# Bucket numbers in HBM for the attention masks of a three-stage kernel

## What is computed

```python
B, H, S, D = 2, 8, 768, 64
q_bits = (einsum('bhsd,dk->bhsk', q, proj) > 0)       # 6 bits, k likewise
q_bucket = sum(q_bits * 2 ** arange(6), axis=-1)
mask = q_bucket[:, :, :, None] == k_bucket[:, :, None, :]
scores = where(mask, scale * q @ k.T, -1e9)
attn = exp(scores - max(scores))
attn = attn / (sum(attn, axis=-1, keepdims=True) + 1e-09)
out = attn @ v
```

## Time and profile before

| | us |
|---|---|
| median of three runs | 756.55 |
| lowest, highest | 755.89, 757.7 |
| the profiled execution, its own time | 757.69 |
| its span in the trace | 755.9 |
| TensorE busy | 713.7 |
| VectorE busy | 440.0 |
| ScalarE busy | 321.3 |
| GpSimd busy | 265.3 |

### The profile page before, as it was taken

How to read it: one execution, slowest core, us unless ns; L and a number is a source line. 1 busy time by engine, 2 the same in 40 slices (tenths; PEclk the granted TensorE clock), 3 DMA queues, 4 the chain that set the end, 5 groups by cost and what they waited for, 6 DMA issues and landing times.

```text
span 755.9 us, 12025 instructions
## 1 busy us (share of the span) xinstructions
PE 713.7 (94%) x3809; PEld 594.4 (79%) x3809; DVE 440.0 (58%) x794; ACT 321.3 (43%) x634; POOL 265.3 (35%) x269
## 2 busy tenths in 40 slices
PE   5989999999999999999999999999983999999995
PEld 2478888888888987888888888888872788778883
DVE  0399999999999966547446555643438421331110
ACT  0077777787787854221222222222313322443221
POOL 1646667667667751007004401700001121112121
PEclk9999999999999999999999999999995999999998
DMA  9821321321233030001100200010116620101010
GB/s 275 255 63 54 95 63 52 93 64 52 56 87 125 1 112 0 1 2 55 56 1 6 105 0 0 1 55 1 56 57 242 230 86 29 56 28 57 28 57 32
DMA packets 22348, 50.80 MB, mean 67 GB/s; under 512 B 3136, under 2 KB 5312, under 8 KB 22304
## 3 DMA queue, kind: packets, MB, share of 16 engines
q1 hardware_dynamic: 19008, 42.34, 17.5%
q0 software_dynamic: 2320, 7.34, 2.9%
q10 hardware_dynamic: 976, 0.56, 0.4%
HBM read 43.95 MB, written 6.55 MB: 67 GB/s over the span
## 4 chain that ended last, share of the span: by engine, by line
PE 85%; DVE 6%; issue 3%; DMA 3%; ACT 1%; SPq 1%; DVEq 0%; POOL 0%; ACTq 0%; POOLq 0%
PE ps L1188 8%; PE ps L1207 7%; PE ps L1352 6%; PE ps L1353 6%; PE ps L1354 6%; PE ps L1334 6%; PE ps L1336 6%; PE ps L1335 6%; PE ps L1221 4%; PE ps L1222 4%; PE ps L1463 3%; PE ps L1465 3%; PE ps L1464 3%; PE ps L1423 3%; PE ps L1425 3%
## 5 line engine op out<-in xcount | busy, mean ns | idle before, releaser
L612 ACT ACTIVATE probs<-ps,neg_max 128x768 f32<-128x768 f32 x96 | 87.0, 907 | 56.0 <-DVE neg_max L821 55.7
L676 ACT ACTIVATE relu<-ps 128x512 f32<-128x512 f32 x48 | 28.7, 598 | 190.5 <-PE ps L1336 190.5
L830 DVE TENSOR_TENSOR pt_lo<-ps,pt_hi 128x384 fp32r<-128x384 f32 x192 | 98.5, 546 | 5.0 <-ACT pt_hi L623 3.0
L623 ACT ACTIVATE pt_hi<-ps 128x384 fp32r<-128x384 f32 x192 | 86.4, 498 | 25.2 <-PE ps L1207 15.1
L1207 PE MATMUL ps<-cst,probs 128*128 128x128 f32 x576 | 92.1, 276 | 1.9 <-DVE pt_lo L830 1.2
L821 DVE TENSOR_REDUCE neg_max<-ps 128x1 f32<-128x768 f32 x96 | 90.5, 944 | 0.0
L1207 PEld LDWEIGHTS ps<-cst,probs 128*128 128x128 f32 x576 | 69.5, 144 | 10.2 <-DVE pt_lo L830 6.7
L1352 PE MATMUL ps<-wo_hi,g_hi 128*128 128x512 f32 x192 | 76.1, 396 | 0.7 <-DVE xt_lo L898 0.7
L1353 PE MATMUL ps<-wo_lo,g_hi 128*128 128x512 f32 x192 | 75.4, 393 | 0.0
L1354 PE MATMUL ps<-wo_hi,g_lo 128*128 128x512 f32 x192 | 75.4, 393 | 0.0
L1334 PE MATMUL ps<-xt_hi,wi_hi 128*128 128x512 f32 x192 | 75.1, 391 | 0.0
(11 more groups left out here) (155 smaller groups left out, 1531.1 us busy)
## 6 DMA issues: line engine op xcount, KB each, us to landing
w_raw<-w SPq DMA_DIRECT2D x16, 512.0 KB, 5.6
raw_k<-kT SPq DMA_DIRECT2D x32, 192.0 KB, 3.2
raw_q<-qT SPq DMA_DIRECT2D x32, 192.0 KB, 3.5
wi_raw<-w_in SPq DMA_DIRECT2D x4, 1024.0 KB, 5.0
wo_raw<-w_out SPq DMA_DIRECT2D x4, 1024.0 KB, 5.2
pair_raw<-qT SPq DMA_DIRECT2D x8, 384.0 KB, 9.0
pair_raw<-kT SPq DMA_DIRECT2D x8, 384.0 KB, 14.7
raw_v<-v SPq DMA_DIRECT2D x16, 192.0 KB, 2.4
```

What stands on the lines that cost most here:

```text
L830: nc.vector.tensor_tensor(pt_lo[c % 2][sl], unit(tt, h).rearrange("p (k q) -> p k q", k=3), pt_hi[c % 2][sl].bitcast(F32), ALU.subtract).t ...
```

## The change

The bucket numbers themselves are now made once and kept in HBM. At the start TensorE multiplies `bits` with the powers of two (`powers`, made on VectorE from the patterns and a row of indices by seven small operations, `prepare`) for three column ranges of q and of k; VectorE copies the results to `bucket_ids` with a factor 1/32 (the patterns sum gives 32 for each one bit's weight); SyncE writes them with three stores to the HBM tensor `buckets`, waits for these, and goes on to its loop.

In the loop a transfer for each head broadcasts the head's q and k numbers to 64 partitions of `bucket_of`, issued between that head's q and k loads and its v load. At tile 4 of each pair but the last, VectorE makes all masks of the next pair with one comparison of `bucket_of` with the partition's own number (`lane`), which gives 1 or 0 for q and for k. It waits for both transfers of the next pair and until `mask_st` has been read. The matmuls and comparisons beside tiles 2, 3, 5, 6, 8 and 9 are gone. GpSimd copies the q half as before and turns 1 and 0 of the k half into 0 and −2^60 on the way. Pair 0 gets its masks as before.

`row_sum` gets a second column that holds 1e-9, and `add_eps` becomes a reduction over the two columns.

```diff
-MASK_TILES = (2, 3, 5, 6, 8, 9)
-MASK_UNITS = len(MASK_TILES)
+MASK_UNITS = 6
+MASK_TILE = 4
+ID_ROWS = 32
...
+    buckets = nc.dram_tensor("buckets", (NH, 2, SEQ), BF16).ap()
...
-        row_sum = sb("row_sum", [P, CHUNKS_PER_PAIR, CHUNK_TILES], F32)
+        row_sum = sb("row_sum", [P, CHUNKS_PER_PAIR, CHUNK_TILES, 2], F32)
...
+            sp.wait_ge(ids_kept, 2)
+            for a in range(3):
+                sp.dma_start(buckets[:, :, MASK_W * a:MASK_W * (a + 1)],
+                             bucket_ids[ID_ROWS * a:ID_ROWS * a + NH, :, :]).then_inc(ids_out, 16)
+            sp.wait_ge(ids_out, 48)
+
+            def load_buckets(i, z):
+
+                sp.wait_ge(masks_staged, i + (MASK_UNITS - 1))
+                sp.dma_start(bucket_of[half(z, True), :, :], buckets[ds(i * 2 + z, 1), :, :].to_broadcast(
+                    [HD, 2, SEQ])).then_inc(ids_in, 16)
+
             with sp.Fori(1, PAIRS) as i:
-                load_heads(i, False)
+                for z in range(2):
+                    load_head(i, z, False)
+                    load_buckets(i, z)
+                    load_v(i, z, False)
...
-                pool.wait_ge(masks_staged, i * MASK_UNITS + MASK_UNITS)
+                pool.wait_ge(masks_staged, i + MASK_UNITS)
                 pool.wait_ge(scores_done, i * TILES_PER_PAIR + (QT * (z + 1) - TILES_PER_PAIR))
                 m = half(z, True)
-                for c, stack in ((0, qb), (1, kb)):
-                    copied(stack[z][m, :], mask_st[m, c, :], 1.0, masks_in, i * 4 + (2 * z + c + 1))
+                copied(qb[z][m, :], mask_st[m, 0, :], 1.0, masks_in, i * 4 + (2 * z + 1))
+                hold()
+                G.tensor_scalar(kb[z][m, :], mask_st[m, 1, :], 1.0, BIG, ALU.subtract,
+                                ALU.mult).then_inc(masks_in, 1)
+                pool.wait_ge(masks_in, i * 4 + (2 * z + 2))
...
-                if tt in MASK_TILES and not last:
-
+                if tt == MASK_TILE and not last:
+
+                    v_.wait_ge(ids_in, i * 32 + 32)
                     v_.wait_ge(masks_in, i * 4 + 4)
-                    m = MASK_TILES.index(tt)
-                    stage_mask(m, slice(0, P), mask_st[:, m // 3, :], beside(z, MASK_W)).then_inc(masks_staged, 1)
+                    nc.vector.tensor_scalar(mask_st[:, :, :], bucket_of[:, :, :], lane[:, :], None,
+                                            ALU.is_equal).then_inc(masks_staged, 1)
...
-                nc.vector.tensor_scalar(row_eps[:, c, :], row_sum[:, c, :], 1e-9, None, ALU.add).then_inc(eps_done, 1)
+                nc.vector.tensor_reduce(row_eps[:, c, :], row_sum[:, c, :, :], AX, ALU.add).then_inc(eps_done, 1)
...
+            def keep_ids(c):
+                v_.wait_ge(ids_turned, c + 1)
+                nc.vector.tensor_scalar(bucket_ids[:, c, :], ps[0:3 * ID_ROWS, 7 - c, 256:512], 1.0 / 32, None,
+                                        ALU.mult).then_inc(ids_kept, 1)
+
             for c, stack in ((0, qb), (1, kb)):
                 units = range(3 * c, 3 * c + 3)
                 for m in units:
                     keep_bits(m)
+                keep_ids(c)
...
+                pe.wait_ge(prepared, 5)
+                for a in range(3):
+                    last_mm = mm(ps[ID_ROWS * a:ID_ROWS * (a + 1), 7 - c, 256:512], powers[:, :],
+                                 bits[:, c, MASK_W * a:MASK_W * (a + 1)], start=True, stop=True)
+                last_mm.then_inc(ids_turned, 1)
...
-                if tt in MASK_TILES and not last:
-                    last_mm = masks(i + 1, MASK_TILES.index(tt), beside(tt % 2, MASK_W))
```

More of the change, by code:

```diff
@@ L125, in program @@
         mask_st = sb("mask_st", [P, 2, SEQ], BF16, 2)
+        bucket_of = sb("bucket_of", [P, 2, SEQ], BF16, 2)
+        bucket_ids = sb("bucket_ids", [3 * ID_ROWS, 2, MASK_W], BF16, 2)
+        powers = sb("powers", [NH * NBITS, ID_ROWS], BF16, 2)
+        lane_hi = sb("lane_hi", [P, 1], F32)
+        lane = sb("lane", [P, 1], F32)
         raw_q = [sb(f"raw_q{z}", [P, SEQ], F32) for z in range(2)]
@@ L263, in program @@
         masks_staged = sem("masks_staged")
+        prepared = sem("prepared")
+        ids_turned = sem("ids_turned")
+        ids_kept = sem("ids_kept")
+        ids_out = sem("ids_out")
+        ids_in = sem("ids_in")
         masks_in = sem("masks_in")
@@ L380, in load_v @@
                     "a p t d -> (a p) t d")).then_inc(v_in[z], 16)
[L382 to L385, removed]
             load_head(0, 0, True)
@@ L612, in exp @@
                 nc.scalar.activation(probs[z][:, :], score_bank(z), ACT.Exp, bias=neg_max[:, z:z + 1],
-                                     accum_out=row_sum[:, c, j:j + 1]).then_inc(exp_done, 1)
+                                     accum_out=row_sum[:, c, j, 0:1]).then_inc(exp_done, 1)
             def round_units(i, tt, first):
@@ L795, in keep_bits, with first_mask_of @@
                                         ALU.is_gt).then_inc(bits_done, 1)
-            def stage_mask(m, part, dst, src):
+            def first_mask_of(m, part, dst, src):
                 col = MASK_W * (m % 3)
@@ L873, in pair, with prepare @@
                             invert(i - 1, c + CHUNKS_PER_PAIR)
+            def prepare(ins, count):
+                ins.then_inc(prepared, 1)
+                v_.wait_ge(prepared, count)
+            heads = patt[:, :].rearrange("p (h b) -> p h b", b=HD)
+            weighed = x_rows[0:NH * NBITS, 0:2, :, :].rearrange("p a t d -> p (a t d)")[:, 0:NH * HD].rearrange(
+                "p (h b) -> p h b", b=HD)
+            prepare(nc.vector.memset(row_sum[:, :, :, 1], 1e-9), 1)
+            prepare(nc.vector.memset(powers[:, :], 0.0), 2)
+            prepare(nc.vector.tensor_tensor(weighed, heads, iota128[0:NH * NBITS, 0:HD].unsqueeze(1).to_broadcast(
+                [NH * NBITS, NH, HD]), ALU.mult), 3)
+            weights = x_rows[0:NH * NBITS, 2, 0, 0:NH]
+            prepare(nc.vector.tensor_reduce(weights, weighed, AX, ALU.add), 4)
+            prepare(nc.vector.tensor_copy(powers[:, 0:NH], weights), 5)
+            prepare(nc.vector.tensor_scalar(lane_hi[:, :], tokid[:, 0:1], float(HD), -float(HD), ALU.is_gt, ALU.mult), 6)
+            prepare(nc.vector.scalar_tensor_tensor(lane[:, :], tokid[:, 0:1], -1.0, lane_hi[:, :], ALU.add, ALU.add), 7)
+            def keep_ids(c):
+                v_.wait_ge(ids_turned, c + 1)
+                nc.vector.tensor_scalar(bucket_ids[:, c, :], ps[0:3 * ID_ROWS, 7 - c, 256:512], 1.0 / 32, None,
+                                        ALU.mult).then_inc(ids_kept, 1)
             for c, stack in ((0, qb), (1, kb)):
@@ L882, in _ @@
                         v_.wait_ge(masks_turned, m + 1)
-                        placed = stage_mask(m, half(z, True), stack[z], first_mask(m))
+                        placed = first_mask_of(m, half(z, True), stack[z], first_mask(m))
                         if z == 1:
@@ L1135, in _, with masks @@
             mm = nc.tensor.matmul
-            def masks(i, m, dst):
-                return mm(dst, patt[:, ds(i * P, P)],
+            def masks(m, dst):
+                return mm(dst, patt[:, 0:P],
                           bits[:, m // 3, MASK_W * (m % 3):MASK_W * (m % 3) + MASK_W], start=True, stop=True)
@@ L1147, in first_masks @@
                     pe.wait_ge(masks_staged, 2)
+                    pe.wait_ge(ids_kept, 1)
                 for m in range(3 * c, 3 * c + 3):
                     pe.wait_ge(bits_done, m + 1)
-                    masks(0, m, first_mask(m)).then_inc(masks_turned, 1)
+                    masks(m, first_mask(m)).then_inc(masks_turned, 1)
+                pe.wait_ge(prepared, 5)
[3 more added lines that the diff above has]
+                last_mm.then_inc(ids_turned, 1)
             pe.wait_ge(projb_in, 16)
@@ L1172, in turn_back, with scores @@
                 return last_mm
-            def scores(i, tt, first, last):
+            def scores(i, tt, first):
                 z, j = divmod(tt, QT)
@@ L1236, in pair @@
                     if tt < TILES_PER_PAIR - 2:
-                        scores(i, tt + 2, first, last_)
+                        scores(i, tt + 2, first)
                     elif not last_:
-                        scores(i + 1, tt + 2 - TILES_PER_PAIR, False, False)
+                        scores(i + 1, tt + 2 - TILES_PER_PAIR, False)
                     c, part = divmod(tt - 4, CHUNK_TILES)
@@ L1255, in pair @@
                         turn_xt(1)
-            scores(0, 0, True, False)
-            scores(0, 1, True, False)
+            scores(0, 0, True)
+            scores(0, 1, True)
             pe.wait_ge(masks_staged, MASK_UNITS)
+            pe.wait_ge(ids_kept, 2)
             pair(0, True, False)
```

## The result

The changed kernel takes 832.63 us (median of four runs, 827.3 to 835.77) against 757.11 us: 1.099 times as long, 95% interval 1.093 to 1.106. The forecast was 803 us, at most 822. Direction and place were right, the size was not: the loss is 75.5 us where 46 were forecast. The profiled execution took 830.55 us, its span 828.7 us; from the 757.69 us of before, that is +72.9 us.

A forecast was written before the change was run, and what follows sets the result against it. Attention was taken as bound by two nearly full engines, TensorE and VectorE. Six longer intervals between pairs (+41.5 us), the start (+5.7) and the end (−1.0) gave +46.2 us: 803 us as a median, range 784 to 822.

The forecast's parts named there:

- The loop and its point: Attention, tile 4: VectorE's comparison waits some 6.5 us for bucket transfers queued behind loads that need split_qk's last piece.
- The rival of transfers in time: Attention pairs: second bucket transfer goes out before the z=1 loads, VectorE never waits; 745 us, chance 0.07.
- The rival without a lower clock: Attention pairs: the wait comes, clock stays up, VectorE's relief covers part; 787 to 794 us, chance 0.24.
- T to the end of split_qk: GpSimd, from the pair's split_v start for z=0 (T) to the end of the last kb copy: 11.94 us.
- Loads and transfer: DMA queue, each pair: four z=1 loads issued, then the bucket transfer in 3.3 us; landed at T + 17.9.
- Rival 3: Bucket transfers: 64 descriptors reading the same 3 KB of HBM are slow, 3 us more each; 830 us, chance 0.08.
- The comparison: VectorE at tile 4: one instruction of 1536 bf16 elements per partition takes 1.0 us, bounds 0.5 and 2.6.
- TensorE resumes 1.7 us after the comparison: Tile 4: x_rows 0.25, maximum 0.86, first half of pt_lo with its signal 0.6 precede TensorE's restart.
- To the next T: Attention pair: from TensorE's restart to the next pair's split_v start on GpSimd takes 14.5 us.
- Clock: TensorE after its stop in each pair: half clock costs 1.5 us, bounds 0 and 2.5.
- Sum of a beat: Attention, one pair of heads: 36.6 us against 29.68 before, +41.5 us over six intervals.
- The start: Before and in pair 0: making and storing bucket numbers, then a 3.3 us wait, move the first T by +5.7 us.

## Why the prediction was right or wrong

- *The loop and its point*: right. The wait stands at tile 4, is released by `bucket_of`, and its release hangs on the last piece of `split_qk`. The rival of transfers in time, at 0.07, did not come; with the transfers put first and the cheap copy the time is 748 to 750 us, where that rival had 745. The rival without a lower clock, at 0.24, was wrong too: the clock fell to 0.50 in the pairs.
- *T to the end of split_qk, 11.94 us*: this is the step that failed most. It was read from the kernel before, and on that very stretch lies `place_masks`, whose copy the change rewrites. "One operation of the same size in place of another: nothing" was wrong by 1.95 us (2776 ns for 830); the chain ends at 126.96, T + 13.90. Why this copy is slower stays open.
- *Loads and transfer*: issued 2.76 us later (2.6 given); landing 4.20 us in this pair, 4.0 at the median, for which I gave 3.3 from rows of 3.4. With the copy: landed at T + 20.9, where the upper bound was 19.1, so VectorE stood 10.3 us and not 5 to 7. Rival 3, the slow broadcast read, named 830 us, the measured time, but by luck: it took 3 us more for a transfer, and a median of 4.0 against 3.3 for the loads of k is an excess of 0.7.
- *The comparison*: 1.0 us given; from landing to `x_rows` it took 1.91 us. The bound of 0.5 to 2.6 held. By itself it takes 0.62 us; two of the seven did so, and the two shortest beats, 38.5 and 39.6 us, are theirs. The Trainium skill, "VectorE: DVE Perf Modes", section "The perf-mode tier table", led to an estimate of 0.56 us: the 0.62 us where nothing holds it up is near it. Behind a GpSimd operation, with up to 2.22 us, it does not hold. The Trainium skill, "GPSIMD Engine Reference", section "Key points", says that GpSimd contends with VectorE instructions in a 2-port mode, which would explain it; I had used that sentence for the reduction only.
- *TensorE resumes 1.7 us after the comparison*: 1.73. *To the next T*: 14.5 given, 14.68 at full clock. *Clock*: 1.5 given, 1.7 measured. All three were right.
- *Sum of a beat*: 36.6 given; 36.6 + 1.95 (copy) + 0.15 (issue) + 0.9 (landing) + 0.9 (comparison) + 0.4 (TensorE and its clock) = 40.9, the pair shown. Over six intervals the mean excess is 40.34 − 36.6 = 3.7, so 22.5 us.
- *The start*: first T at 68.0 given, 72.16 measured, +4.2. "`prepare` runs on an idle VectorE" was wrong. It is idle for want of constants, which come at 21.8 us; then the operations run until 26.5 and the first bits wait, at 26.58 us where VectorE began at 23.70 before. The first line here is of the kernel before, the others are of the changed one:

```profile
23.70 1.08 DVE L793 TENSOR_SCALAR bits<-ps 96x256 bf16<-96x256 f32 x3 [23.70 <-PE ps L1161]
...
21.79 0.07 DVE L909 MEMSET row_sum<- 128x12 f32 x1 [21.79 <-DMA mb_sb<-mod_bias]
...
26.58 1.08 DVE L818 TENSOR_SCALAR bits<-ps 96x256 bf16<-96x256 f32 x3
...
54.21 1.70 DVE L839 TENSOR_SCALAR mask_st<-bucket_of,lane 128x1536 bf16<-128x1536 bf16 x1 [5.91 <-issue]
```

  The bits of k come 1.9 us later than before, at 36.20. The last bucket transfer goes out at 49.28 us (46.5 given), and the comparison starts at 54.21 (49.8 given), 4.9 us behind it where 3.3 was given. So of the 4.2 us 2.8 are lost by the issue, of which `prepare` makes 1.9 at most, and 1.6 in the landing; from the comparison's start to T it took 0.2 us less than given.
- *The end*: −1.0 given; from the last T on, 517.4 us before and 516.3 after: right.
- *Together*: 803.9 + 22.5 + 4.2 = 830.6, and the profiled execution took 830.55.
- *The range* was narrowed by the argument that not all terms go to one end. Three of them went up: the copy, the landing and the comparison. Copy and comparison have GpSimd in common. For the landing this is not shown: with the idle matmuls, where GpSimd stands still, a transfer still took 3.87 us to the comparison (127.31 to 131.18), where 3.3 was given. The bounds were also added up wrongly: with start and end as given, 34.4 to 39.2 us make 791 to 820 and not 784 to 822. Even the full upper bound of 40.4 makes 827 us, below the measured time, for want of the copy and the start.

## What to carry to other kernels

Before a transfer is hung into a queue in order, ask what the loads ahead of it wait for; a prefetch for the next round that stands behind a load which needs this round's work is no prefetch. When a change turns a side chain into the path, price again every operation on that chain, the ones that look like a change of operands too. And take the pieces of a mixed change one by one: here the smallest, a reduction over two columns, alone gave as much as all of them together.

## What the runs showed of the hardware

- GpSimd's `tensor_scalar` on 64 × 768 elements takes 0.83 us with multiply and multiply, and 2.77 us with subtract and multiply or multiply and subtract, in forms that also have 2^60 as a scalar. I had not expected a difference.
- Two VectorE `tensor_scalar` operations from SBUF to SBUF are prolonged by GpSimd operations that run when they start: 0.62 to 2.22 us for the same comparison, and 0.15 to 1.78 us for three elements. The reduction of two columns never was (142 to 152 ns in 32 instances), nor were the mask comparisons out of PSUM in the kernel before (467 to 484 ns in 42).
- Which of the two pays depends on who starts first: GpSimd's two-input operation took 2.18 us instead of 1.80 where the comparison had started 0.1 us before it. So the price is a matter of phase: a slower GpSimd copy halved the mean `row_eps`.
